# Attention's first batch rescheduled: q and k turned in the value banks, the score ring kept for blocks, and the first pair of heads scored without stacked operands

## The reference, cut to what matters

```python
scores = scale * np.matmul(q, k.transpose(0, 1, 3, 2))      # q, k, v: 4 x 8 x 576 x 64
thresh = np.max(scores, axis=-1, keepdims=True) - tau
scores = np.where(scores >= thresh, scores, -1000000000.0)
attn = np.exp(scores - np.max(scores, axis=-1, keepdims=True))
attn = attn / (np.sum(attn, axis=-1, keepdims=True) + 1e-09)
x = np.matmul(attn, v)                                       # then to 4 x 576 x 512
# _moe_ref: u = x + (x^T U V)^T ; x = u + relu(u @ w_ch1) @ w_ch2
# _moe2_ref: each row goes to one of 8 experts (512 -> 1024 -> 512), times its gate
```

## Time and profile before

| | us |
|---|---|
| runs shown | 1200.15, 1206.53, 1209.03 |
| their median | 1206.53 |
| the profiled execution's own time | 1202.22 |
| its span, first to last instruction | 1199.7 |
| first block scored, at | 21.54 |
| last transpose of a block of the first batch, at | 137.13 |
| PE busy over the span | 1084.5 (90%) |
| DVE, ACT, POOL busy | 587.6, 438.0, 345.5 |

### The profile page before, as it was taken

How to read it: one execution, slowest core, us unless ns; L and a number is a source line. 1 busy time by engine, 2 the same in 40 slices (tenths; PEclk the granted TensorE clock), 3 DMA queues, 4 the chain that set the end, 5 groups by cost and what they waited for, 6 DMA issues and landing times. The chain is left out here.

```text
span 1199.7 us, 20063 instructions
## 1 busy us (share of the span) xinstructions
PE 1084.5 (90%) x7110; PEld 948.3 (79%) x7111; DVE 587.6 (49%) x1155; ACT 438.0 (37%) x719; POOL 345.5 (29%) x322
## 2 busy tenths in 40 slices
PE   3677789999999999998999989899947999999996
PEld 2555579989978989997998989699946788788785
DVE  1366555575545655655566653222248335254641
ACT  1355453333344434335433322311143334244531
POOL 2355103254330533541054424044211112112111
PEclk9999999999999999998999989899966999999998
DMA  6666503252442424336052311122056345153611
GB/s 147 148 164 161 121 1 89 86 155 63 119 134 62 120 73 127 109 92 168 17 148 62 101 54 44 66 72 71 1 198 205 135 159 184 45 174 121 207 65 37
DMA packets 111449, 129.16 MB, mean 108 GB/s; under 512 B 67373, under 2 KB 67373, under 8 KB 111344
## 3 DMA queue, kind: packets, MB, share of 16 engines
q1 hardware_dynamic: 106160, 116.15, 34.3%
q0 software_dynamic: 3520, 10.75, 2.8%
q10 hardware_dynamic: 1664, 0.89, 0.3%
HBM read 87.90 MB, written 10.22 MB: 82 GB/s over the span
## 5 line engine op out<-in xcount | busy, mean ns | idle before, releaser
L757 ACT ACTIVATE ex<-score_banks,stat 128x576 f32<-128x576 f32 x131 | 97.0, 740 | 206.8 <-DVE stat L855 206.8
L651 PE MATMUL mlp_banks<-u_hi,w_hi 128*128 128x320 f32 (+1 forms) x512 | 158.1, 309 | 7.6 <-DVE hid_lo L914 4.7
L659 PE MATMUL mlp_banks<-hid_hi,w_hi 128*128 128x320 f32 (+1 forms) x512 | 157.6, 308 | 7.7 <-DVE z L922 7.2
L482 POOL TENSOR_TENSOR w_lo<-stage,w_hi 128x1024 fp32r<-128x1024 f32 x64 | 152.7, 2386 | 4.6
L651 PE MATMUL mlp_banks<-u_hi,w_lo 128*128 128x320 f32 (+1 forms) x512 | 152.2, 297 | 0.0
L651 PE MATMUL mlp_banks<-u_lo,w_hi 128*128 128x320 f32 (+1 forms) x512 | 152.1, 297 | 0.0
L659 PE MATMUL mlp_banks<-hid_hi,w_lo 128*128 128x320 f32 (+1 forms) x512 | 151.4, 296 | 0.0
L659 PE MATMUL mlp_banks<-hid_lo,w_hi 128*128 128x320 f32 (+1 forms) x512 | 151.3, 295 | 0.0
L478 POOL CAST w_hi<-stage 128x1024 fp32r<-128x1024 f32 x64 | 66.5, 1038 | 269.9 <-PE mlp_banks L651 231.9
L865 DVE SCALAR_TENSOR_TENSOR ex<-score_banks,stat,ex 128x576 f32<-128x576 f32 x131 | 106.9, 816 | 60.6 <-ACT ex L757 49.6
L586 PE MATMUL score_banks<-k_tiles,q_tiles 128*128 128x288 f32 x580 | 106.3, 311 | 28.5 <-ACT et_first L767 12.3
(11 more groups left out here) (230 smaller groups left out, 2012.5 us busy)
## 6 DMA issues: line engine op xcount, KB each, us to landing
stage<-in_moe_w_ch SPq DMA_DIRECT2D x64, 512.0 KB, 3.9
w_raw<-in_moe_w SPq DMA_DIRECT2D x64, 512.0 KB, 5.3
q_tiles<-q_parts SPq DMA_DIRECT2D x32, 320.0 KB, 3.9
q_tiles<-q_parts SPq DMA_DIRECT2D x64, 160.0 KB, 4.2
k_tiles<-k_parts SPq DMA_DIRECT2D x60, 144.0 KB, 3.5
raw_q<-in_q SPq DMA_DIRECT2D x32, 128.0 KB, 2.4
raw_v<-in_v SPq DMA_DIRECT2D x32, 128.0 KB, 2.7
raw_k<-in_k SPq DMA_DIRECT2D x30, 128.0 KB, 2.8
```

Of the source, the lines that this page charges most:

```text
L482: nc.gpsimd.tensor_tensor(w_lo[:, n % RING], stage[:, n % 2], w_hi[:, n % RING].bitcast(F32), ALU.subtract).then_inc(w_split, 1)
L651: last = nc.tensor.matmul(bank[:, 0:w], ch1(a, g, d, c), of[:, d, cols], start=(d == 0 and n == 0), stop=(d == KC - 1 and n == 2))
L659: last = nc.tensor.matmul(bank[:, 0:w], ch2(a, g, q, c), of[:, q, 0:w], start=(q == 0 and n == 0), stop=(q == QUARTER - 1 and n == 2))
L757: nc.scalar.activation(ex_of(n), score_of(n), ACT.Exp, bias=stat[:, n % 4, 0:1], scale=-1.0).then_inc(exp_done, 1)
```

## The change

- Three-slot ring: only blocks. Block n uses slot n modulo 3, and `scores(n+3)` follows `turn(n)` when `et_copied` has reached n+1.
- q and k of pair p+2 are turned into `aux` in parts while pair p runs: the last rows of both ("tails", two transposes) after block 2, the four full pieces of q after block 3, those of k after block 6. Each has its own copy on ACT. `raw_q` and `raw_k` have two buffers, and loads run one pair further ahead.
- Values: two chunks of products after a block (2, 2, 1) where it was 2 and 3, or 3 and 2. `turn_out` of the first half comes after block 7 of the same pair, and its `write_x` in block 8; `inverse` is made in two parts.
- Pair 0: scored from `first_q` (laid over `u_lo`) and `first_k` (over `u_hi`), written by ACT and DVE directly from the turned q and k. `first_k` has zeros in the other head's 64 rows, so that no stacking is needed, and scoring takes 3 passes (6 products a block, 12 for the ninth). POOL clears two pieces of 64x1152 first.
- ACT issues the loads of k for pairs 0 and 1; SP issues q of both at once. POOL's v4 work goes to block 6 of pairs 1, 2 and 3; the gate weights are loaded in pair 1.
- From n = 36 on the parts are the same and their order too, except that q and k are loaded one pair earlier and v one step later.

```diff
-def lead_order():
-    seq = [("q", 0), ("k", 0), ("q", 1), ("k", 1)]
...
+LATER = PAIRS_OF + 2
+QUEUED = 3
...
+    first_q = u_lo[:].rearrange("p a b -> p (a b)")[:, 0:2 * PAD].rearrange("p (t n) -> p t n", t=2)
+    first_k = u_hi
...
+    def bank_of(n):
+        slot = n % 3 if n < ALONE else n % 2
+        return mlp_banks[:] if slot == 2 else score_banks[:, slot]
...
+    def part_bank(p, part):
+        at = 512 if part == "k" and p < LATER else 0
+        return aux[:, at:at + 512]
...  SP
         issue_q(sp, 0)
-        sp.wait_ge(q_turned, 1)
         issue_q(sp, 1)
-        sp.wait_ge(k_turned, 1)
-        issue_k(sp, 1)
-        stack_q(0)
         load_v(0)
+        load_q_and_k(2)
         stack_q(1)
         stack_k(1)
...  POOL
-                if p == 0 and j in (2, 3, 4):
-                    spread_v(j - 2, n + 1)
+                if p and j == 6:
+                    spread_v(p - 1, n + 1)
+                if j == 4:
+                    upper_q(p + 2)
                 if j == 5:
-                    upper_q(p + 2)
-                if j == 6:
                     low_q(p + 2)
...  PE
+        def first_scores(n):
+            p, j, h, i = place(n)
+            if j == 0:
+                pe.wait_ge(first_k_low, 1)
+                pe.wait_ge(first_q_low, 1)
+                pe.wait_ge(cleared, PADS + 3)
+            if j == 1:
+                pe.wait_ge(first_k_low, 2)
+            of = [h] if j < STEPS - 1 else [0, 1]
+            for a in range(2):
+                for m in of:
+                    for t, (q_part, k_part) in enumerate(((0, 0), (0, 1), (1, 0))):
+                        last = nc.tensor.matmul(score_of(n)[:, a], first_q[:, q_part, i * P:(i + 1) * P], first_k[:, 2 * m + k_part, a * HALF:(a + 1) * HALF],
+                                                start=(m == of[0] and t == 0), stop=(m == of[-1] and t == 2))
+            last.then_inc(scored, 1)
...
+        first_turns()
+        turn_part(1, "q")
+        turn_part(1, "k")
+        scores(0)
+        turn_part(1, "tails")
+        scores(1)
+        scores(2)
+        for n in range(ALONE):
+            p, j, _, _ = place(n)
+            turn(n)
+            if p and j < 3:
+                values(p - 1, 1, ((0, 1), (2, 3), (4,))[j])
+            if j == 2:
+                turn_part(p + 2, "tails")
+            if p and j == 3:
+                turn_out(p - 1, 1)
+            if j == 3:
+                turn_part(p + 2, "q")
+            if 4 <= j < 7:
+                values(p, 0, ((0, 1), (2, 3), (4,))[j - 4])
+            if j == 6:
+                turn_part(p + 2, "k")
+            if j == 7:
+                turn_out(p, 0)
+            if n + QUEUED < ALONE + 2:
+                pe.wait_ge(et_copied, n + 1)
+                scores(n + QUEUED)
...  ACT
+        for n in range(ALONE):
+            p, j, _, _ = place(n)
+            copy_turned(n)
+            exponentials(n + 2)
+            if p and j == 2:
+                copy_out(p - 1, 1)
+            if j == 2:
+                copy_part(p + 2, "tails")
+            if j == 3:
+                copy_part(p + 2, "q")
+            if j == 6:
+                copy_out(p, 0)
+                copy_part(p + 2, "k")
...  DVE
+        for n in range(ALONE):
+            p, j, _, _ = place(n)
+            if p and j == 4:
+                write_x(p - 1, 1)
+            if j == 8:
+                write_x(p, 0)
+            mask(n)
+            minimum(n + 2)
+            if p and j == 2:
+                inverse(p - 1, 4, 2 * NT)
+            if j == 6:
+                inverse(p, 0, 4)
```

More of the change, by code:

```diff
@@ L460, in upper_k @@
         def upper_k(p):
-            cols_ready(p, k_copied)
-            pool.wait_ge(k_stacked, K_STACK * p)
+            pool.wait_ge(part_copied, max(part_count(p, "k"), part_count(p, "tails")))
+            if p >= 2:
+                pool.wait_ge(k_stacked, K_STACK * (p - 1))
             nc.gpsimd.tensor_copy(k_parts[:, 0], k_cols[:]).then_inc(k_upper, 1)
@@ new lines, in k_piece, with first_turns @@
+        def k_piece(p, c):
+            return raw_k[:, p % 2, c].rearrange("p a d -> p (a d)")
+        def first_turns():
+            pe.wait_ge(q_loaded[0], Q_DMAS)
+            for c in range(NT):
+                last = nc.tensor.transpose(score_banks[:, 0, c * P:(c + 1) * P], q_piece(0, c), ident[:])
+            last.then_inc(first_turned, 1)
+            pe.wait_ge(k_loaded[0], K_DMAS)
+            for c in range(NT):
+                last = nc.tensor.transpose(score_banks[:, 1, c * P:(c + 1) * P], k_piece(0, c), ident[:])
+            last.then_inc(first_turned, 1)
@@ new lines, in turn_part @@
+        def turn_part(p, part):
+            to = part_bank(p, part)
+            if part != "k":
+                pe.wait_ge(q_loaded[p % 2], Q_DMAS * (p // 2 + 1))
+            if part != "q":
+                pe.wait_ge(k_loaded[p % 2], K_DMAS * (p // 2 + 1))
+            if p == 1:
+                if part == "tails":
+                    pe.wait_ge(part_copied, part_count(1, "q"))
+            elif p >= LATER:
+                if part == "q":
+                    pe.wait_ge(x_written, 2 * (p - 1) - 1)
+                else:
+                    pe.wait_ge(part_copied, part_count(p, part) - 1)
+            elif part == "q":
+                pe.wait_ge(part_copied, part_count(p, "tails"))
+            elif p == 2:
+                pe.wait_ge(part_copied, part_count(1, part))
+            else:
+                pe.wait_ge(x_written, 2 * (p - 2) - (1 if part == "tails" else 0))
+            if part == "tails":
+                nc.tensor.transpose(to[:, 0:P], q_piece(p, NT - 1), ident[:])
+                last = nc.tensor.transpose(to[:, P:2 * P], k_piece(p, NT - 1), ident[:])
+            else:
+                for c in range(NT - 1):
+                    last = nc.tensor.transpose(to[:, c * P:(c + 1) * P], q_piece(p, c) if part == "q" else k_piece(p, c), ident[:])
+            last.then_inc(part_turned, 1)
@@ L833, in _ @@
                 copy_out(p - 1, 1)
-            if LED <= p + 1 < PAIRS and j < 3:
-                copy_part(p + 1, j)
+            if LATER <= p + 1 < PAIRS and j < 3:
+                copy_part(p + 1, ("q", "k", "tails")[j])
             if j == 4 and p < PAIRS:
```

324 lines of the change are left out of this document (109 added, 215 removed).

## The result

| | before | after |
|---|---|---|
| median of the runs, us | 1205.15 (4 runs) | 1187.05 (4 runs, 1182.86 to 1193.75) |
| ratio after / before | | 0.985, 95% interval 0.981 to 0.989 |
| the profiled execution | 1202.22 | 1193.75 |
| its span | 1199.7 | 1192.0 |
| granted clock over it | 0.968 | 0.953 |

The forecast was 1174: the time is inside the range, 1163 to 1188, but little over half of the 32.4 us came.

What follows compares the result with a forecast made beforehand. Before 137 us PE was held by stacking, V's late cast, its lower clock and ring waits. 16.4 + 23.5 + 3 x 22.3 - 2.1 = 104.7 against 137.13, 32.4 us less: 1174 us, range 1163 to 1188.

Steps and rivals of the forecast that it cites:

- The start: Up to the first turn: block 0 scored at 10.2 us, 11.3 earlier; first turn at 16.4 in place of 28.46.
- The clock: PE's dense work from about 8 to 16 us brings the higher clock, taken as holding from there on.
- Rival 1: Late rise of PE's clock, with dense work again in blocks 3 to 5: 7.8 us lost, time 1182; 22%.
- Pair 0: First pair's nine blocks at the higher clock: 22.3 us plus 1.2 for DVE's and ACT's extras, 23.5.
- Steady pairs: Pairs 1 to 3: 22.3 us each in place of 25.55, with 1.6 allowed for turns held back.
- Rival 2: The ring gives nothing: pairs stay at 25.5 us, 3 x 3.2 lost, time 1184; 14%.
- Pair 1: Second pair: taken as a steady pair of 22.3 us, its q and k stacked in time by a margin of 2 us.
- rival 4: Late stack of pair 1 and late first weight piece take back all but 10 us of the gain; 3%.
- The MLP's PE-bound stages shift as a whole: nothing: After the first batch: the MLP's stages move earlier as a whole, at no gain or loss.
- The sum: Last turn of the first batch at 104.7 us against 137.13, so 32.4 us less.

Runs made afterwards that it cites:

- stacked_first: The changed kernel, but pair 0 goes through operands stacked by DMAs as before the change; median 1195.10 us, ratio 0.991 to the kernel before.
- piece_early: The changed kernel, but SP issues the first two weight pieces right after the load of pair 1's v; median 1183.40 us.
- v_step1: The changed kernel, but from the second batch on v is loaded behind block 1 again, not block 2; median 1179.84 us, ratio 0.979.
- before_v2: The kernel before, but from the second batch on v is loaded behind block 2, not block 1; median 1214.05 us against 1206.56, ratio 1.006.
- again: The changed kernel with nothing altered, run and profiled a second time; median 1184.58 us, ratio 0.982 to the kernel before.
- quarters: The changed kernel, but POOL's split of each weight piece is four instructions of 256 columns, not one of 1024; median 1162.81 us, ratio 0.965.

## Why the prediction was right, and where it was short

- **The start**: block 0 scored at 10.59 (forecast 10.2), first turn at 15.89 (16.4), in place of 28.46. Right, by its own steps.
- **The clock**: up at 14 us, inside the 8 to 16 named. Rival 1 is out. The reason, dense work ahead of it, agrees with stacked_first (3.65 us of 4 busy for 2.60 before); no run varies it alone.
- **Pair 0**: 23.0 us (15.89 to 38.87), forecast 23.5.
- **Steady pairs**: 22.7 for pair 2, 21.0 from the turn at 90.28 to the last, which is pair 3 less one block's loop, forecast 22.3 and 20.2. Rival 2 is out.
- **Pair 1: the step that failed first.** It took 28.7 for 22.3; beside pair 2, 2.7 us of the excess are idle time of PE and the rest is the lower clock. It is the wait named in rival 4, "a first weight piece that SP issues later than POOL wants it", and dismissed with "No place in the rows has room for that much". The batch ended 30 us sooner by the forecast, and POOL wants the piece that much sooner, but its issue stayed behind SP's other loads. The prediction followed ten stacking issues past SP, and not the 22 issues that stood between them and the piece, from 24.06 to 38.07. The run piece_early gives 5.7 back in pair 1.
- **"The MLP's PE-bound stages shift as a whole: nothing": the step that failed second.** It left out POOL's splits beside DVE altogether. The price was 11 to 15 us from pair 4 to 15. The move of v's load by one block was in the description of the change and got no term. It is 6.6 of it by v_step1 (550.4 against the mean of 559.3 and 554.7), 8.5 by before_v2 (552.5 against 544.0). Of either, 5 to 6 are idle time of PE, and the rest is the clock. What is left is in pair 4 (up to 4, the MLP's first products, L640, at the lower clock in the first trace, not in "again") and in other falls of the clock that move from trace to trace.
- **The sum.** 32.4 less 6.6 by the last turn is 25.8; the medians say 18.1. The two traces say 7.7 and 14.8 at the end, of 25.8 and 27.5 at the last turn, so the sum closes only within the spread of the traces. With both loads placed as said, the last turn is at 105.22 for 104.7: the terms of the first stretch were sized rightly. That the time, 1172.53, also meets the 1174 is partly luck. In its trace the stretch from pair 4 to 15 still takes 548.7 for 544.0, and the price "nothing" for it holds only where POOL's splits are short (534.0 and 534.5).

**Open**: how much of the 5.7 us that the early pieces win in their stretch reaches the end. The medians give 1.2 alone, 7.3 beside v_step1 (1179.84 to 1172.53) and 1.4 beside quarters (1162.81 to 1161.40), each with some 4 to 7 us to either side. And what decides the falls of the clock that follow no long wait: they stand at other places in "again" than in the first trace.

## What to carry to other kernels

A load that is moved shifts every load behind it on its queue, and what then changes is which engines run at the same time: follow the queue to the next engine that wants its data. Where DVE has tiny SBUF instructions on the path, keep GpSimd's instructions short; look at the longest duration of such a group, not at its mean. And an edit that makes one stretch faster can make the first transfer of the next one late.

## What the runs showed that was not expected

- DVE's 128x1 sum, median 160 ns, took up to 2307 ns beside POOL's 128x1024 split of 2383 ns. Before, 28 limits and inverses of over 0.9 us made 45 us of DVE time; cutting them short, to 3 such rows there and 2 in the changed kernel, is worth 17.7 us and 21.8. DVE's masks never exceeded 821 ns in v_step1, whatever POOL did.
- Four splits of 256 columns take 2.94 us where one of 1024 takes 2.38, so some 0.19 us more for each further instruction.
- The same program's profiled spans differ by 7 us (1192.0 and 1184.9), with PE's lows at other places.
